# Two mixtures of experts behind local attention: h written to memory in the order in which it is read back

## What is computed

```python
for e in range(E):                      # first mixture: once for each of the token's two experts
    h = np.maximum(x[mask] @ w1[e], 0.0)        # 512 -> 1024
    out[mask] += top2_w[mask, k, None] * (h @ w2[e])   # 1024 -> 512
...
    h = np.maximum(xe @ w1[e], 0.0)     # second mixture, one expert a token
    ye = h @ w2[e]
    out[mask] = gate_w[mask, None] * ye
```

## Time and profile before

| | us |
|---|---|
| runs | 1156.57, 1158.09, 1162.10; median 1158.09 |
| the profiled execution, its own time | 1158.69 |
| its span in the profile | 1156.6 |
| TensorE busy | 1085.6 (94%) |
| VectorE busy | 643.4 (56%) |
| ScalarE busy | 280.0 (24%) |
| GpSimd busy | 317.1 (27%) |
| first mixture, roughly | from 130 to 760 |
| second mixture, roughly | from 820 to 1150 |

### The profile page before, as it was taken

One profiled execution on the slowest core, in us unless ns is written; L12 is line 12 of the kernel. 1 busy time (PEld: TensorE's weight loads), 2 busy tenths in 40 slices (PEclk: granted clock), 3 DMA queues, 4 the chain that ended last, 5 costly groups with the idle time before them and its releaser, 6 DMA issues.

```text
span 1156.6 us, 29685 instructions
## 1 busy us (share of the span) xinstructions
PE 1085.6 (94%) x7939; PEld 879.6 (76%) x7940; DVE 643.4 (56%) x1360; ACT 280.0 (24%) x534; POOL 317.1 (27%) x473
## 2 busy tenths in 40 slices
PE   5989788999999999999999999989889999999995
PEld 4767566788888888888888888856668888878783
DVE  2767585655553552644635536317885246576861
ACT  3566321121212212121212122115211212121111
POOL 2004313332222232333322223220133223333321
PEclk9797889999999999999999999999999999999998
DMA  8998974877685774766867757559387447777952
GB/s 344 357 336 282 329 247 131 242 219 220 184 234 138 216 209 137 221 198 162 244 168 204 222 131 215 137 114 252 100 280 230 141 157 236 236 244 234 306 178 68
DMA packets 126990, 245.87 MB, mean 213 GB/s; under 512 B 17454, under 2 KB 70878, under 8 KB 126960
## 3 DMA queue, kind: packets, MB, share of 16 engines
q1 hardware_dynamic: 48608, 112.38, 28.9%
q10 hardware_dynamic: 61728, 90.25, 24.1%
q0 software_dynamic: 16624, 42.88, 16.7%
HBM read 169.51 MB, written 76.73 MB: 213 GB/s over the span
## 4 chain that ended last, share of the span: by engine, by line
PE 63%; DVE 7%; DMA 6%; issue 5%; DVEq 4%; ACT 1%; ACTq 1%; POOL 1%; POOLq 0%
PE moe_ps_y L1597 10%; PE moe_ps_y L1598 10%; PE moe_ps_y L1602 10%; PE moe_ps_h L1597 10%; PE moe_ps_h L1598 9%; PE moe_ps_h L1602 9%; DMA moe_h_moved<-h_d 3%; PE moe_ps_x L1590 3%; DVE weights L141 2%; DVEq L1478 2%; DMA moe_xg<-x_d,moe_from_row 2%; ACTq L1660 1%; DVE moe_h_lo L1710 1%; DVEq L141 1%; PE g_bank L343 1%
## 5 line engine op out<-in xcount | busy, mean ns | idle before, releaser
L1597 PE MATMUL moe_ps_h<-weights,moe_x_hi 128*128 (+1 forms) x640 | 253.1, 395 | 11.8 <-ACT moe_x_hi L1665 4.9
L1597 PE MATMUL moe_ps_y<-weights,moe_h_hi 128*128 (+1 forms) x624 | 251.5, 403 | 7.0 <-ACT moe_y L1685 3.4
L1598 PE MATMUL moe_ps_h<-weights,moe_x_hi 128*128 (+1 forms) x640 | 251.0, 392 | 0.0
L1598 PE MATMUL moe_ps_y<-weights,moe_h_hi 128*128 (+1 forms) x624 | 244.6, 392 | 0.0
L1710 DVE SCALAR_TENSOR_TENSOR moe_h_lo<-moe_h_moved,moe_h_hi 128x256 fp32r<-128x256 f32 x312 | 111.8, 422 | 231.2 <-ACT moe_h_hi L1674 231.2
L1674 ACT ACTIVATE moe_h_hi<-moe_h_moved 128x1024 fp32r<-128x1024 f32 x78 | 82.8, 1062 | 383.5 <-PE moe_ps_y L1602 313.9
L1602 PE MATMUL moe_ps_h<-weights,moe_x_lo 128*128 (+1 forms) x640 | 171.7, 390 | 0.0
L147 DVE TENSOR_TENSOR weights<-stage,weights (+1 forms) x128 | 156.8, 1225 | 19.7 <-DVE weights L141 19.2
L1602 PE MATMUL moe_ps_y<-weights,moe_h_lo 128*128 (+1 forms) x624 | 154.1, 389 | 0.0
L1597 PEld LDWEIGHTS moe_ps_h<-weights,moe_x_hi 128*128 128x128 f32 x640 | 121.2, 189 | 41.8 <-issue 15.3
L1597 PEld LDWEIGHTS moe_ps_y<-weights,moe_h_hi 128*128 128x128 f32 x624 | 117.8, 189 | 32.4 <-issue 7.1
(11 more groups left out here) (259 smaller groups left out, 861.8 us busy)
## 6 DMA issues: line engine op xcount, KB each, us to landing
stage<-in_w SPq DMA_DIRECT2D x128, 512.0 KB
h_d<-moe_h_turned ACTq DMA_DIRECT2D x80, 512.0 KB
moe_h_moved<-h_d ACTq DMA_DIRECT2D x320, 128.0 KB
v_sb<-in_v SPq DMA_DIRECT2D x24, 520.0 KB, 5.3
k_sb<-in_k SPq DMA_DIRECT2D x24, 512.0 KB, 6.3
x_d<-zero SPq DMA_DIRECT2D x27, 260.0 KB, 7.2
q_sb<-in_q SPq DMA_DIRECT2D x24, 256.0 KB, 4.5
x_d<-x_sb ACTq DMA_DIRECT2D x24, 256.0 KB, 6.0
```

Source lines behind the costliest of these rows:

```text
L1597: pe.matmul(out, a_hi, b_hi, start=(i == 0), stop=False)
L1598: pe.matmul(out, a_hi, b_lo, start=False, stop=False)
```

## The change

`h_d` holds rows in the order of the reader: row b*32 + p, columns a*256 to a*256 + 255 hold what partition a*32 + p of `h_turned` has for block b. `park` makes four transfers, one for each b: the source is 128 partitions x 1 KB, the destination is 4 blocks (a) of 32 rows (p) of 1 KB. The first two wait for the first half's turn alone, the last two for both. `fetch` makes one transfer, 128 rows of 4 KB on both sides. The counts that `moved` and `parked` are compared with follow.

```diff
-        self.h_blocks = h_d.rearrange("(a p) (b r) -> b p a r", a=QB, b=QB)
+        self.h_parts = [h_d[b * QR:(b + 1) * QR, :].rearrange("p (a r) -> a p r", a=QB) for b in range(QB)]
...
     def park(self, act, t):
 
         s = self.s
-        act.wait_ge(s("turned"), t * 2 + 4)
         if not (isinstance(t, int) and t == 0):
-            act.wait_ge(s("moved"), t * (16 * QB))
-        act.dma_start(self.h_d, self.h_turned[:, :, :, :].rearrange("p b c q -> p (b c q)")).then_inc(s("parked"), 16)
+            act.wait_ge(s("moved"), t * 16)
+        for f in range(2):
+            act.wait_ge(s("turned"), t * 2 + (f + 3))
+            for b in (2 * f, 2 * f + 1):
+                act.dma_start(self.h_parts[b], self.h_turned[:, b, :, :].rearrange("p c q -> p (c q)"))\
+                   .then_inc(s("parked"), 16)
 
     def fetch(self, act, t):
 
         s = self.s
-        act.wait_ge(s("parked"), t * 16 + 16)
+        act.wait_ge(s("parked"), t * (16 * QB) + 16 * QB)
         if not (isinstance(t, int) and t == 0):
             act.wait_ge(s("h_split"), t)
-        for b in range(QB):
-            act.dma_start(self.h_moved[b * QR:(b + 1) * QR, :, :, :].rearrange("p a c q -> p a (c q)"),
-                          self.h_blocks[b]).then_inc(s("moved"), 16)
+        act.dma_start(self.h_moved[:, :, :, :].rearrange("p a c q -> p (a c q)"), self.h_d).then_inc(s("moved"), 16)
...
-        act.wait_ge(s("moved"), t * (16 * QB) + 16 * QB)
+        act.wait_ge(s("moved"), t * 16 + 16)
...
-            dve.wait_ge(s("parked"), t * 16)
+            dve.wait_ge(s("parked"), t * (16 * QB))
```

## The result

| | before | after |
|---|---|---|
| median of four runs each, us | 1157.33 | 1378.76 |
| lowest and highest, us | 1155.15, 1162.10 | 1374.13, 1389.08 |
| ratio, 95% interval | | 1.1919 (1.1874 to 1.1964) |
| span of the profiled execution, us | 1156.6 | 1372.2 |

The change makes the kernel 19% slower. The forecast was 1290 us in a range of 1170 to 1390; the median measured lies 11 us under the upper end of that range.

What follows compares the result with a forecast made beforehand. The prediction took TensorE to bound the first mixture, with park and fetch hidden under 11.35 us a tile. Adding +92, +37, +7 and +2 us to 1158.7 gave 1297, put at 1290 us, range 1170 to 1390.

Steps and rivals of the forecast that it cites:

- The park runs on four engines: Each new park, with outermost count 4 in memory, gets 4 DMA engines, not 16; ScalarE's queue falls to 57888 packets.
- The park: Writing h to memory on four engines: 1.34 us fixed plus 6.55 us of data at 20.0 bytes a ns, 7.89 us.
- The fetch: Reading h back as one transfer of 128 rows of 4 KB, priced as the old park: 2.63 us for 4.33.
- What others add: Other queues hold each engine 4.46 us per tile; partly filling gaps, they lengthen the turn from 10.52 to 13.2 us.
- The sum: Both mixtures, bare round trips and tail add 138 us to 1158.7, making 1297, put at 1290 for tiles with less competition.
- my two lines: Loss by mixture: first, 50 tiles x (13.2 - 11.35) = +92 us; second, 23 tiles x (13.2 - 11.6) = +37 us.
- bare round trips: Two at the second mixture's start, each park +5.3 us and each fetch -1.7 us: +7 us together.
- The early half brings nothing: Two parks waiting for the first turn alone gain nothing in the loop; without ScalarE's cover, at most 1.33 us.
- Rival A: Parks still run on sixteen engines; second mixture gains 6 us, tail 2, bare round trips 0.6: about 1151 us, chance 0.12.
- rival C: Sixteen engines, but 1.4 us more issues ahead of the high part of h eat the gain: 1155 to 1160 us, chance 0.04.
- Rival B: Four engines, but a turn of 9.13 us stays hidden in 11.35; only bare places pay: 1168 to 1180 us, chance 0.07.
- The lower clock: Risk of more time: TensorE, waiting in every tile, may be granted its lower level, 1.2 GHz, for part of it.

Runs made afterwards that it cites:

- e1_rows32: The changed kernel with each park taking one group of 32 partitions with its four blocks, and the early start dropped: 1161.9 us, ratio 1.0021.
- e2_pad: The kernel before with h_d padded to 33 rows for each 32, so its one park has outermost count 4: 1586.8 us, ratio 1.3693.
- e4_four: The kernel before with its one park cut into four transfers of 32 rows of 4 KB: 1176.8 us, ratio 1.0145.

## Why the prediction was right

- **The park runs on four engines.** Right, and shown from both sides: 57888 packets, to the last one as forecast, and two edits that switch it (e1_rows32 off, e2_pad on). The sentence of the Trainium skill (DMA: Bandwidth & Descriptors, section on why a DMA increments its semaphore by 16), that the number is the largest up to 16 that divides the slowest dimension of both sides, agrees with every count of closing packets here: 4 for 128 and 4, 2 for 64 and 2, 16 for 32 and 32. That the four parks share the same engines follows from the 7.9 us that they take together; had they lain on four different groups of four, each group would have had a quarter of it. The prediction took this step from that page alone and priced no case in which they do not meet.
- **The park**, forecast 7.89 us: 7.87 in the tile above and 7.91 alone (961.22 to 969.13). The size is right, its reason was luck. 7.89 has the 20.0 bytes a ns of a loaded engine; for an engine alone the prediction had 25.4, so 6.50 us. But the park alone moved 128 KB on each engine in 6.6 us, 19.9 bytes a ns, with next to nothing beside it, and the parks of the loop without weight packets take no longer, though gathers and scatters run beside them. Load is not what makes it slow; what does stays open.
- **The fetch**, forecast 2.63 us at its least, priced as a park: the shortest in the loop is 3.24 us and the bare one of e1_rows32 3.20. A transfer that reads memory was priced by one that writes it, 0.6 us too low. In the first bare round trip of the second mixture, where 1.7 us were to come back on the fetch, it takes 4.75 us beside a weight piece and a gather: nothing came back.
- **What others add**, forecast 13.2 - 10.52 = 2.7 us of their 4.46: what is left of the measured tile is 13.93 - 7.87 - 3.24 = 2.8. As a mean that is right in the first mixture; in the second it is 3.2 us, and I had taken the same. The picture of gaps that others' packets fill evenly was not right: the parks grow by nothing in 34 of 48 tiles and by 0.6 to 8 us in the 14 in which weights arrive.
- **The sum** is therefore short by the term of the turn, 13.2 for 13.93 and 14.29: with the measured turns my two lines would have read 50 x 2.58 = 129 us for 92 and 23 x 2.69 = 62 us for 37, which is 62 of the 78 us by which the spans' 215.6 pass my sum of 138. The rest lies mostly in the passage between the mixtures, 21.5 us with the four tiles behind it, of which I had 7 as bare round trips. Forecast +132 us, measured +221: the direction and the cause were right, the size was short by two fifths, and the 7 us taken off the 1297 for tiles with less competition went the wrong way.
- **The early half brings nothing.** Right, but in the changed kernel not for the reason given, that ScalarE's queue stands at the high part of x. In the tile whose parks go out at 608.46 the high part of x is over at 605.53, and both turns at 605.74, which began only behind the landing of the park before; the parks go out when the fetch has landed, 2.7 us later. From VectorE's timeline:

```profile
604.43 1.31 DVE L1702 STREAM_TRANSPOSE moe_h_turned<-moe_ps_h 128x512 f32<-128x512 f32 x2 [3.24 <-DMA h_d<-moe_h_turned]
```

- **Rival A** (full width, 1151 us) was the right counterpart and wrong in size: at full width the layout is worth 0.2% of loss, not 0.6% of gain, because, as rival C had it, the issues cost about as much as the fetch gives back (e4_four, +1.5%). **Rival B** is out: its turn of 9.13 us needed 25.4 bytes a ns, and even a turn without weight packets takes 12.6.
- The lower clock is a consequence that was named as a risk. In the chain that ended last TensorE has 8%, so it cost little; no run took it alone.

## What to carry to other kernels

Before a transfer is cut or turned around, look at the outermost count on both sides: in every run here that, not the bytes, said how many DMA engines a transfer from ScalarE's queue gets, and a 4 there makes a park of 512 KB take 7.9 us for 2.6. Count the closing packets of a queue to see it. Then ask whether the transfer stands in a chain with one buffer: here a second h_d gave back 98 of 221 us with the parks as narrow as they were, and full width gave back all. And one long transfer in place of four short ones pays only if the four short ones do not come back on the other side: here three more issues on a queue that carries compute cost about as much as three fewer saved.

## What was not expected of the hardware

- On four engines a park of 128 rows of 4 KB takes 10.05 us alone, four parks with 512 runs of 1 KB 7.9 us; on sixteen engines it is the other way round, 2.63 and 3.7 us (1.78 of these are the four issues). What is behind it stays open.
- An issue of a narrow transfer is slower: 0.53 us in the median for outermost 4, four in a row or a single one (e2_pad), against 0.46 for four of 32 rows and 0.34 for one of 128. With outermost 2 the median is 0.52, and the longest of them take up to 4.7 us. From the trace of the changed kernel, then of e1_rows32 (the instructions that touch h_d: duration in ns, least, median, most):

```profile
L1653 ACTq DMA_DIRECT2D h_d<-moe_h_turned x320: 512/530/1647, 152.4 to 1341.4; - x160
```

```profile
L1652 ACTq DMA_DIRECT2D h_d<-moe_h_turned x320: 309/458/1058, 154.8 to 1132.5; - x160
```
